# Loads by need, weight halves apart and a first dense product in two halves: the opening of a kernel of linear attention and two dense layers

## The reference

```python
# q, k, v: (4, 8, 768, 64) f32
gamma = 1.0 - 2.0 ** (-5.0 - np.arange(H))
for t in range(S):
    state = gamma * state + outer(k[:, :, t], v[:, :, t])      # per batch and head, 64 x 64
    y[:, :, t] = (1 / sqrt(D)) * q[:, :, t] @ state
x = y as (3072, 512)
# first dense layer pair, d_ff 2048
h = x @ w_in
g = np.where(h >= 1, h, np.where(h <= -1, 0.0, (h + 1) ** 2 / 4))
x = g @ w_out
# second dense layer pair, d_ff 1024
h = x @ w_in2;  solu = h * softmax(h);  ln = layernorm(solu) * g_ln
out = ln @ w_out2
```

## Time and profile before

| | |
|---|---|
| Median of 3 runs | 891.05 us (891.0 to 892.11) |
| The profiled execution | 890.45 us |
| Its span | 888.7 us |
| Granted clock over the span | 1.0 |
| TensorE busy | 873.4 us, 98% |
| VectorE, ScalarE, POOL busy | 46%, 32%, 24% |
| HBM read and written | 56.9 MB, 25.2 MB |

### The profile page before, as it was taken

The page is one execution under the profiler, slowest core; times in us unless marked ns, Lnnn a source line. Parts: engine busy times, 40 slices in busy tenths (PEclk is TensorE's granted clock), DMA queues, the critical chain, the costliest instruction groups (busy, mean ns, idle before and its releaser), DMA issues.

```text
span 888.7 us, 11899 instructions
## 1 busy us (share of the span) xinstructions
PE 873.4 (98%) x4864; PEld 719.5 (81%) x4864; DVE 411.9 (46%) x666; ACT 283.0 (32%) x438; POOL 211.6 (24%) x185
## 2 busy tenths in 40 slices
PE   6999999999999999999999999999999999999997
PEld 5788888888888888888888888888888888888886
DVE  5544443333433343333433343443566666666662
ACT  2333342122312232122322133334334444444442
POOL 2555432223222323223222112226100000000000
PEclk9999999999999999999999999999999999999999
DMA  9912102111111111211101104300444444444443
GB/s 347 340 49 69 63 4 92 48 48 48 48 60 48 48 36 66 76 50 36 48 36 36 36 1 166 119 1 0 143 131 146 156 149 142 145 152 150 158 133 104
DMA packets 50742, 82.84 MB, mean 93 GB/s; under 512 B 5248, under 2 KB 23680, under 8 KB 50688
## 3 DMA queue, kind: packets, MB, share of 16 engines
q1 hardware_dynamic: 50400, 81.56, 27.0%
q10 hardware_dynamic: 288, 0.53, 0.2%
HBM read 56.90 MB, written 25.17 MB: 92 GB/s over the span
## 4 chain that ended last, share of the span: by engine, by line
PE 67%; DVE 18%; issue 5%; ACT 4%; DMA 3%; POOL 2%; SPq 1%; POOLq 0%; ACTq 0%; DVEq 0%
PE acc L342 30%; PE h L329 29%; DVE solu L804 3%; DVE zq L819 3%; ACT e L755 3%; DVE h_max L794 3%; DVE zT_lo L785 3%; PE att L270 2%; PE att L283 2%; DVE z L815 2%; PE att L286 2%; POOL rstd L832 1%; DVE x_lo L777 1%; DMA mask<-in_mask 1%; PE att L299 1%
## 5 line engine op out<-in xcount | busy, mean ns | idle before, releaser
L342 PE MATMUL acc<-g_hi,w 128*128 128x512 f32 x768 | 256.8, 395 | 0.0
L329 PE MATMUL h<-x_hi,w 128*128 128x512 f32 x768 | 252.4, 390 | 3.6 <-DVE x_lo L458 2.1
L608 POOL TENSOR_TENSOR g_lo<-g_raw,g_hi 128x512 fp32r<-128x512 f32 x96 | 123.4, 1285 | 404.5 <-ACT g_hi L369 404.5
L418 ACT ACTIVATE g_raw<-g_raw,half_bias 128x512 f32<-128x512 f32 x96 | 69.5, 724 | 347.6 <-DVE g_raw L543 347.6
L329 PEld LDWEIGHTS h<-x_hi,w 128*128 128x128 f32 x768 | 144.2, 188 | 34.0 <-ACT x_hi L369 2.4
L342 PEld LDWEIGHTS acc<-g_hi,w 128*128 128x128 f32 x768 | 144.1, 188 | 33.1 <-issue 0.7
L543 DVE TENSOR_SCALAR g_raw<-h 128x512 f32<-128x512 f32 x96 | 66.4, 691 | 185.1 <-PE acc L342 184.3
L342 PE MATMUL acc<-g_lo,w 128*128 128x512 f32 x384 | 149.8, 390 | 0.0
L329 PE MATMUL h<-x_lo,w 128*128 128x512 f32 x384 | 149.4, 389 | 0.0
L548 DVE TENSOR_TENSOR g_raw<-h,g_raw 128x512 f32<-128x512 f32 x96 | 66.4, 692 | 62.3 <-ACT g_raw L418 61.7
L329 PEld LDWEIGHTS h<-x_lo,w 128*128 128x128 f32 x384 | 72.1, 188 | 14.9
(11 more groups left out here) (69 smaller groups left out, 872.6 us busy)
## 6 DMA issues: line engine op xcount, KB each, us to landing
z<-zq SPq DMA_DIRECT2D x24, 512.0 KB, 2.6
zt<-z SPq DMA_DIRECT2D x96, 128.0 KB, 2.9
kT<-in_kT SPq DMA_DIRECT2D x24, 256.0 KB, 2.7
q<-in_q SPq DMA_DIRECT2D x24, 256.0 KB, 2.7
v<-in_v SPq DMA_DIRECT2D x24, 256.0 KB, 2.9
x2T<-y SPq DMA_DIRECT2D x24, 256.0 KB, 2.6
x_raw<-x2T SPq DMA_DIRECT2D x12, 512.0 KB, 4.3
out<-o SPq DMA_DIRECT2D x24, 256.0 KB, 2.0
```

What stands on the lines that cost most here:

```text
L329: last = mm(hb[f % 2][:, :], ww, xx[:, kt, :], start=kt == 0 and t == 0, stop=kt == KT - 1 and t == 2)
L342: last = mm(acc[m][:, :], ww, gg[:, f % 2, :], start=f == 0 and t == 0, stop=f == FT1 - 1 and t == 2)
L418: nc.scalar.activation(gate[:, f % 2, :], gate[:, f % 2, :], ACT.Square, bias=half_bias[:, 0:1], scale=0.5).then_inc(sem["squared"], 1)
L608: tt(g[1][:, f % 2, :], gate[:, f % 2, :], g[0][:, f % 2, :].bitcast(F32), ALU.subtract)\
```

## The change

SP's loads come in another order: the first mask third, v of a chunk two loads of kT and q later, the in halves of the weights ahead of the out halves, which are loaded singly later. `split_weights` on ScalarE becomes two functions with semaphores of their own; the out half of slice f is now split in step f of block 0, by ScalarE and POOL, and the in half of slice f + 3 in the same step. TensorE runs three matmuls on a zeroed tile first, then the outputs of chunk c directly behind the scores of chunk c + 2. The first product, `first_up`, is done in two halves of 256 columns with its passes outermost, so 24 matmuls, and POOL makes the lo part of its weights. The updates of chunks 0 to 3 move two slots later. VectorE's waits for `mask` and `tables` move to the first use of each.

```diff
-W_READY = 2
+W_READY = 3
+WARM_UP = 3
+FIRST_UPDATE = 2
...
-            def load_weights(f):
+            def load_w_in(f):
                 sp.dma_start(w_raw[f][:, 1, :], io["moe_w_in"][f]).then_inc(sem["w_in_loaded"][f], 16)
+
+            def load_w_out(f):
                 sp.dma_start(w_raw[f][:, 3, :], io["moe_w_out"][f]).then_inc(sem["w_out_loaded"][f], 16)
...
             for c in range(B):
                 load("kT", c)
                 load("q", c)
-            for c in range(2):
-                load("v", c)
-            load_weights(0)
+                if c == 0:
+                    sp.dma_start(mem["first_mask"][:, :, :, :].rearrange("p e a t -> p (e a t)"), io["first_mask"])\
+                        .then_inc(sem["first_mask"], 16)
+                if c >= 2:
+                    load("v", c - 2)
+            load_w_in(0)
             for c in range(2, B):
                 load("v", c)
-            load_weights(1)
+            for f in range(1, W_READY):
+                load_w_in(f)
             sp.dma_start(tables[:, :], io["tables"]).then_inc(sem["tables"], 16)
             for c in range(B):
                 load("kn", c)
-            load_weights(2)
+                if c == 1:
+                    load_w_in(W_READY)
+            load_w_out(0)
+            load_w_in(W_READY + 1)
+            load_w_out(1)
             sp.dma_start(mem["mask"][:, :, :, :].rearrange("p e a t -> p (e a t)"), io["mask"])\
                 .then_inc(sem["mask_loaded"], 16)
             load_chunk(B)
-            for f in range(3, FIRST_PIECE):
-                load_weights(f)
+            for f in range(2, FIRST_PIECE):
+                if f + W_READY < FIRST_PIECE:
+                    load_w_in(f + W_READY)
+                load_w_out(f)
...
             def attention(j, slot):
-                if j == 1 and slot < B:
-                    update(slot)
+                if j == 1 and 0 <= slot - FIRST_UPDATE < B:
+                    update(slot - FIRST_UPDATE)
...
+            def first_up():
+
+                for b in (0, 2):
+                    xs = slice(b * P, (b + 2) * P)
+                    pe.wait_ge(sem["x0_hi"], b + 2)
+                    if b == 0:
+                        pe.wait_ge(sem["w_in_hi"], 1)
+                    for t, (wn, xn) in enumerate(((0, 0), (1, 0), (0, 1))):
+                        if t == 1:
+                            pe.wait_ge(sem["w0_in_lo"], 1)
+                        if t == 2:
+                            pe.wait_ge(sem["x0_lo"], b + 2)
+                        for kt in range(KT):
+                            last = mm(hb[0][:, xs], w[0][:, wn, kt * P:(kt + 1) * P], x[xn][:, kt, xs],
+                                      start=t == 0 and kt == 0, stop=t == 2 and kt == KT - 1)
                 last.then_inc(sem["h_ready"], 1)
...
+            pe.wait_ge(sem["warm"], 1)
+            for n in range(WARM_UP):
+                mm(acc[KT - 1][:, 0:2 * P], mem["warm"][:, 0:P], mem["warm"][:, :], start=True, stop=True)
+            scores(0)
+            scores(1)
             for c in range(B):
-                scores(c)
-            for c in range(B):
+                if c + 2 < B:
+                    scores(c + 2)
                 outputs(c)
...
-                    if blk == 0 and f + W_READY < FT1:
-                        split_weights(f + W_READY)
+                    if blk == 0:
+                        if f + W_READY < FT1:
+                            split_w_in(f + W_READY)
+                        split_w_out(f)
...
-            for c in range(B - 1):
+            first_split(0)
+            split_w_in(0)
+            for c in range(1, B):
                 first_split(c)
-            split_weights(0)
-            first_split(B - 1)
             for f in range(1, W_READY):
-                split_weights(f)
+                split_w_in(f)
...
+                if c == B:
+                    dve.wait_ge(sem["mask_loaded"], 16)
...
+                if c == B:
+                    dve.wait_ge(sem["tables"], 16)
...
+            nc.vector.memset(mem["warm"][:, :], 0.0).then_inc(sem["warm"], 1)
...
-            for c in range(B - 1):
+            for c in range(B):
                 first_split(c)
-            split_weights(0)
-            first_split(B - 1)
             for f in range(1, W_READY):
                 split_weights(f)
-            dve.wait_ge(sem["tables"], 16)
-            dve.wait_ge(sem["mask_loaded"], 16)
             dve.wait_ge(sem["gains"], 16)
...
-                    if blk == 0 and f + W_READY < FT1:
-                        split_weights(f + W_READY)
+                    if blk == 0:
+                        split_weights(f)
...
-            for f in range(W_READY):
-                split_weights(f)
+            pool.wait_ge(sem["w_in_hi"], 1)
+            tt(w[0][:, 1, :], w_raw[0][:, 1, :], w[0][:, 0, :].bitcast(F32), ALU.subtract)\
+                .then_inc(sem["w0_in_lo"], 1)
             pool.wait_ge(sem["tables"], 16)
             for c in range(B):
                 scale_kn(c)
```

More of the change, by code:

```diff
@@ L93, in place @@
     plain("half_bias", [P, 1])
-    plain("warm", [P, 1])
+    plain("scratch", [P, 1])
+    plain("warm", [P, BLK // 2])
     for name in STATISTICS:
@@ L317, in up @@
                 n = blk * FT1 + f
-                if n == 0:
-                    pe.wait_ge(sem["x0_hi"], B)
-                    pe.wait_ge(sem["x0_lo"], B)
                 wait(pe, sem["gmax"], n - 1)
                 if blk == 0:
-                    wait(pe, sem["w_in_lo"], f + 1)
+                    wait(pe, sem["w_in_lo"], f)
                 for kt in range(KT):
@@ L330, in up @@
                                   stop=kt == KT - 1 and t == 2)
+                last.then_inc(sem["h_ready"], 1)
+            def first_up():
[12 more added lines that the diff above has]
+                                      start=t == 0 and kt == 0, stop=t == 2 and kt == KT - 1)
                 last.then_inc(sem["h_ready"], 1)
@@ L347, in dense @@
                 for f in range(FT1):
-                    up(blk, f)
+                    if blk == 0 and f == 0:
+                        first_up()
+                    else:
+                        up(blk, f)
                     if blk < BLOCKS - 1:
@@ L373, in first_split, with split_w_in, split_w_out @@
                 copy(x[0][:, :, c * P:(c + 1) * P], by_pair(y_bank(c))).then_inc(sem["x0_hi"], 1)
-            def split_weights(f):
+            def split_w_in(f):
                 act.wait_ge(sem["w_in_loaded"][f], 16)
+                copy(w[f][:, 0, :], w_raw[f][:, 1, :]).then_inc(sem["w_in_hi"], 1)
+            def split_w_out(f):
                 act.wait_ge(sem["w_out_loaded"][f], 16)
-                copy(w[f][:, 0::2, :], w_raw[f][:, 1::2, :]).then_inc(sem["w_hi"], 1)
+                copy(w[f][:, 2, :], w_raw[f][:, 3, :]).then_inc(sem["w_out_hi"], 1)
             def split_y(blk):
@@ L421, in dense @@
                     copy(g[0][:, f % 2, :], gate[:, f % 2, :]).then_inc(sem["g_hi"], 1)
-                    if blk == 0 and f + W_READY < FT1:
-                        split_weights(f + W_READY)
+                    if blk == 0:
+                        if f + W_READY < FT1:
+                            split_w_in(f + W_READY)
+                        split_w_out(f)
                     if blk == BLOCKS - 1:
                         prepare(f)
-            act.dma_start(mem["first_mask"][:, :, :, :].rearrange("p e a t -> p (e a t)"), io["first_mask"])\
-                .then_inc(sem["first_mask"], 16)
             act.dma_start(mem["g_ln"][:, :], io["g_ln_col"]).then_inc(sem["gains"], 16)
             act.wait_ge(sem["half_set"], 1)
-            nc.scalar.activation(mem["warm"][:, :], half_bias[:, :], ACT.Copy)
-            for c in range(B - 1):
+            nc.scalar.activation(mem["scratch"][:, :], half_bias[:, :], ACT.Copy)
+            first_split(0)
+            split_w_in(0)
+            for c in range(1, B):
                 first_split(c)
-            split_weights(0)
-            first_split(B - 1)
             for f in range(1, W_READY):
-                split_weights(f)
+                split_w_in(f)
             for blk in range(BLOCKS):
@@ L486, in attention @@
             def attention(j, slot):
-                if j == 1 and slot < B:
-                    add_update(slot)
+                if j == 1 and 0 <= slot - FIRST_UPDATE < B:
+                    add_update(slot - FIRST_UPDATE)
                 for c, stage in at_slot(j, slot, STAGES):
@@ L492, in split_weights @@
             def split_weights(f):
-                dve.wait_ge(sem["w_hi"], f + 1)
+                dve.wait_ge(sem["w_in_hi"], f + 1)
                 tt(w[f][:, 1, :], w_raw[f][:, 1, :], w[f][:, 0, :].bitcast(F32), ALU.subtract)\
@@ L597, in split_weights @@
             def split_weights(f):
-                pool.wait_ge(sem["w_hi"], f + 1)
+                pool.wait_ge(sem["w_out_hi"], f + 1)
```

(3 more changed lines are left out.)

## The result

The changed kernel takes 887.97 us in the median of 8 runs (886.81 to 889.49), against 891.15 for the kernel before (889.83 to 892.11, 8 runs). The ratio is 0.9966, 95% interval 0.9956 to 0.9975: faster by 3.2 us, 0.34%. The forecast was 885.0 with a range up to 887.8; the direction was right, the gain was half of what was forecast, and the time lies 0.2 us above the range. The profiled execution took 887.16, its span is 885.4, 3.3 less than before.

A forecast was written before the change was run, and what follows sets the result against it. TensorE, busy 98% of the span, was taken as the bound, full only from 28.56 us. Moving that to 21.6, less 0.94 for two later updates, gave 6.0: 890.45 to 884.45, plus 0.6, 885.0; range 883.9 to 887.8.

The forecast's parts named there:

- The point at 28.56: Start of `up(0, 2)` in the kernel before, from which TensorE is full; forecast to move to 21.6 us.
- the thinnest cover: POOL's out half of w0 done at 24.4, ahead of `down(0, 0)` due at 24.8: 0.4 us to spare.
- the lower estimate of 2.7: First product's 24 matmuls: 2.7 us instead of 3.1 if a weight load takes an estimated 107 ns.
- the weight loads: Rival: first product bound by weight loads, 4.5 us instead of 3.1, giving 886.4; chance 0.12.
- the late wait of each step: Rival: out half of w(f), now split in step f, comes late in 16 steps; 901 at 4.0 each; chance 0.03.
- the second, the low clock: Rival: low clock holds through the opening scores, 1.9 each; 1.1 us lost, 886.1; chance 0.10.
- the fourth, late landings: Rival: loads or POOL's chain up to 3 us late, TensorE waits for `down(0, 0)`; 887.6 at worst; chance 0.12.
- the sixth: Rival: no change, gain handed back by an unseen wait, for instance at the change of phase; 891; chance 0.03.
- a gain of 6.8: Gain at the low end: half price for the first product, outputs 3 ready with v3 at 14.3.
- the forecast's 6.0 us: Shift of TensorE's full point: `up(0, 2)` from 28.56 to 21.6, less 0.94 for two updates put behind it.
- priced at 0.94: Two updates moved behind the start of `up(0, 2)`, 0.47 us each.
- two copies instead of one: ScalarE in later steps: about 1.2 us for 1.06 before, claimed hidden.

The follow-up runs named there:

- e10: Changed kernel with out halves split earlier, updates 2 and 3 side by side, first mask on ScalarE's queue, seven warm-ups, one fill: 884.94 us, ratio 0.9939.
- e15: Kernel before the change, with seven warm-up matmuls ahead of scores 0: 890.35 us, ratio 0.9998.
- e6: Changed kernel with the first dense product in one piece, 12 matmuls of 512 columns: 891.88 us, ratio 1.0008.
- e1: Changed kernel with five more matmuls on the zeroed tile between scores 0 and scores 1: 886.78 us, ratio 0.9953.
- e3: Changed kernel with the first mask's load back on ScalarE's queue: 887.14 us, ratio 0.9959.
- e13: Changed kernel with g_ln's small load moved behind the inputs of chunk 4: 888.65 us, ratio 0.998.
- e12: Changed kernel with the fill behind scores 0 and all scores ahead of all outputs: 888.73 us, ratio 0.9973.
- e7: Changed kernel with updates 2 and 3 side by side behind the first down product: 887.85 us, ratio 0.9966.
- e5: Changed kernel with out halves of the weights split earlier, so none is left for steps 14 and 15: 887.41 us, ratio 0.9958.
- e2: Changed kernel without its three warm-up matmuls: 888.66 us, ratio 0.9973.
- e8: Kernel before the change, with only VectorE's waits for mask and tables moved to their first use: 889.81 us, ratio 0.9994.
- e4: Changed kernel with all four scores ahead of all four outputs: 887.38 us, ratio 0.996.

## Why the prediction was wrong, by its steps

The point at 28.56 and what had to move to bring it forward were read rightly: `mask`, VectorE's line behind it and the paired halves are out of the chain, and no wait stands between 10 and 118 us. The first product (3.1, measured 3.06; its weight loads took 190 ns each and lay under the matmuls, so the lower estimate of 2.7 from a shorter load did not come true), `up(0, 1)` and the first two updates were sized rightly, and POOL was not late for `down(0, 0)`, the thinnest cover, though that product came 2.3 later than forecast and so had more of it (e10 has the 0.4 us as planned). Of the rivals, the weight loads fell, the late wait of each step fell too, and the second, the low clock, came true beside the fourth, late landings. I had given them 0.10 and 0.12, each alone. A wait that I did not see, the sixth, came true in part, at the change of block. The ends of the range do not quite follow from their terms (a gain of 6.8 gives 884.3, not 883.9; the worst late landing gives 887.6, not 887.8); nothing hangs on that.

At `up(0, 2)` 2.0 of the forecast's 6.0 us were missing. Two steps failed.

1. "I take the high level from the second scores on; loads, not TensorE, set the pace there anyway." I judged the gap behind scores 0 by the gap of 2.1 us in the earlier trace rows, which the clock had survived; the new gap was 2.4 us, with TensorE busy for only a part of the time before it, and the clock fell. One gap survived was no evidence: in e15 the same gap of 2.14, behind 14 us in which TensorE stood still for 0.8 in all, let it fall, and so did one of 2.27 in e6, behind more than 170 us without a stop. And TensorE did set the pace: once q1 is there, the chain holds nothing else. e1, which takes only this away, gains 1.55 at `up(0, 2)`. The 1.1 us of the rival was the right kind of price and somewhat small. With the clock held 0.4 of the 2.0 us is left (22.02 in e1 for 21.6).
2. "The first mask moves from ScalarE's queue to third on SP's; it is the same four units, so about 5.9." It landed at 6.7, q1 at 8.0 for 7.3. With the mask on its old queue q1 lands at 7.7 (e3) and 7.3 (e10), and e3 gains 0.37 at `up(0, 2)`; e13 shows that g_ln's pieces are not the reason. But e12 has q1 at 7.1 with the mask on SP's queue, so the queue is not the whole of it, and the cause stays open.

Then 0.6 us was lost on updates 2 and 3, which the forecast priced at 0.94: `up(0, 2)` to the end of `down(0, 1)` took 14.1 us against 12.6 before. A lone update costs 0.62 and makes the next product 2.94 instead of 2.72. e7 gets 0.37 back.

The last term was missing altogether. "In later steps ScalarE pays two copies instead of one (1.06 before, about 1.2 now), hidden" held for all steps but 14 and 15, in which the kernel before had no split and which lie right at the split of x for the next block. Between the end of `down(0, 1)`, 3.5 us earlier than before, and that of the first product of the second block (120.76 against 123.44, 2.7 earlier) 0.8 us went. e5 removes it. By its rows it was less ScalarE's copy than POOL's subtraction, beside which one of VectorE's took 1.77 us and not 0.68; the forecast priced POOL's subtractions by POOL's own time alone. The forecast looked for waits in the first 30 us and for slack in the middle of the block, not at its end.

Together 6.0 - 2.0 - 0.6 - 0.8 = 2.6; the spans differ by 3.3, since the two waits at the change of phase and before the last product were 0.5 shorter in this execution; some 0.2 is unexplained. These are sums over one profile of each kernel.

That e10 comes to 884.94, the forecast's number, is not its proof. It starts `up(0, 2)` at 22.3, not at 21.6, and has the three repairs that the forecast did not know it needed; that the number is the same is luck.

## What to carry to other kernels

When a chain is freed of its loads, what was covered sets the pace: here matmuls at the lower clock, which cost nothing in the kernel before (e15) and 1.5 us after the change (e1). Warm-ups keep little of their worth if a gap follows before the work that they are for (0.65 us with a gap of 2.4 us behind them in the changed kernel, 1.55 more with the gap filled); price the idle time behind them, and fill it. That the clock lived through a gap once does not say that it will again. And a piece of work that is put off within a block has to end somewhere: look at the last steps, where the next block's preparation runs on the same engines.

## What the runs showed of the hardware

- The granted clock reads 1.00 over the opening of the kernel before and of e2, though scores take 2.08 there and 1.16 later in the same stretch; it also reads 1.00 in e12 while the fill takes 4.54 for 2.42. In the changed kernel, whose warm-ups had raised the clock, the same 2.08 reads 0.50. In these profiles the column doesn't show the lower level up to the first change; the length of the instructions does.
- The same gap of 2.14 us before the first product left the clock high in the kernel before and in e8 and let it fall in e15. Behind gaps of 1.92 to 2.18 us in e5, e7 and e13 scores 1 took 1.49, 1.59 and 1.16, between the high level's 1.16 and the low level's 2.08, and scores 2 took 2.05 to 2.08; behind 2.43 in the changed kernel and 2.84 in e4 scores 1 took 2.08.
- Behind the same three warm-ups chunk 0's scores took 1.16 to 1.6 in seven profiles, 1.93 and 1.96 in two, and 2.08 in two (e6 and e12), as if nothing had been raised. Behind seven they took 1.16 in all three profiles.
- The wait before the last product, 1.2 to 2.3 us in every kernel, can also end in a fall of the clock (0.66 from 880 to 885 us in e6), which may be behind the spread of the kernel before as well; that was not tried. In e6's profile it cost 1.5 us.
- VectorE's subtraction of 128x512 from SBUF took 0.68 alone. Where POOL was subtracting when it started, it ended 0.54 to 0.56 us after POOL had ended, as if it had to wait: 0.84 and 1.77 us in the changed kernel (POOL ended at 116.14 and 117.84, VectorE at 116.69 and 118.38), 1.38 in e5 (116.27 and 116.83).
